# Attention in pairs of heads: score products on row halves of the array instead of stacked queries

## The chip, the cores and the metric

The kernel runs on one core of a Trainium2 chip. The metric is the device time of one execution in microseconds, the median of several runs. All stages stand in one program; engines are TensorE (PE in the profile, PEld for its loads of weights), VectorE (DVE), ScalarE (ACT), GpSimd (POOL) and SyncE (SP, which here only issues DMAs).

## The reference

Three stages, the output of each the input of the next: attention with a window of 128 keys and 4 sink keys (4 batches, 8 heads, 768 positions, head size 64); an expert-like layer over 3072 tokens (512 to 2048 to 512, with `h - tanh(h)` between); and a top-1 mixture of eight experts. Cut to the first, which the change is in, and the second, which shares its time:

```python
def _attn_ref(q, k, v, n_sink, window):
    scores = scale * np.matmul(q, k.transpose(0, 1, 3, 2))
    keep = is_sink | in_window
    scores = np.where(keep, scores, -1000000000.0)
    scores = scores - np.max(scores, axis=-1, keepdims=True)
    a = np.exp(scores)
    a = a / (np.sum(a, axis=-1, keepdims=True) + 1e-09)
    return np.matmul(a, v).astype(np.float32)

def _moe_ref(x, w_in, w_out):
    h = x @ w_in
    g = h - np.tanh(h)
    return (g @ w_out).astype(np.float32)
```

## The kernel before

**Tiling.** The 3072 tokens are cut into eight chunks of 384 (`NC`, three blocks of 128 queries, `TPC`). Two chunks are one batch. In a chunk the eight heads are four pairs (`HP`), and a pair of one chunk is a group `g`, 32 in all. A unit is one head and one query block: six in a group, 24 in a chunk, 192 in all. Each float32 operand is split into a float16 high and low part, and products are made of the parts.

**One unit.** `scores` makes two products of 128 rows by 128 queries by 260 keys (previous block, four sinks, own block; 132 in the first block of a batch). The stationary operand is `q_stack`, low queries on partitions 0 to 63 and high ones on 64 to 127; the moving one is first `kl_stack`, then `kh_stack`, which hold the low and high keys twice, on both halves of the partitions. Both accumulate in one bank, `s_ps` (the bank `acc0` for every second unit of the first chunk). VectorE adds the mask and takes the maximum (L585), ScalarE takes exponentials with their sum (L590), VectorE adds and inverts the sum (L602, L603), ScalarE scales (L608, `normed`). `transpose_probs` turns the two 128-column blocks with two transposes of float32 (L645) into one of two banks `pt_ps`; ScalarE takes the high part (L628) and VectorE the low part (L632). After each sixth unit `gather_sinks` and `transpose_sinks` do so for the sink columns of all six. After every second unit `weigh_values` multiplies with the values: the two heads of the pair write partitions 0 to 63 and 64 to 127 of one bank, `x_out`, with products of 64 columns of the array each (L707). After the sixth, `split_x` moves `x_out` into `xt_hi` (ScalarE) and `xt_lo` (VectorE).

**Conversions of a group.** `load_qk` loads each group's queries and keys twice, once to each half of the partitions. `qk_top_of` takes the largest magnitude (VectorE), `qk_scales` works out a power of two from it (eight small instructions, each behind the last), `qk_multiply` scales (GpSimd), `conv` makes the high part (ScalarE) and the low part (GpSimd, VectorE for the first group).

**The order of work** is written out by hand. `alone` runs the first 28 units, with the preparation of the weights beside them (`prepare_alone`). Then come eight windows of 32 slots, one window per chunk. Even slots make the hidden product of the next column block (`mlp_in`, twelve products of 384 columns, into `h_ps`), odd ones the output product (`mlp_out`, nine of 512 columns). ScalarE and VectorE do `tanh` (L762), `mlp_gate` (L771), `mlp_split` (L781) and `mlp_rest` (L791) for it. In each slot that is not a rest, one unit of attention of a later chunk has its scores and the transposes of the unit two before in the middle of the expert products (`between`), and the value products behind them. A product of `mlp_in` waits until `mlp_gate` has read `h_ps`. The router of the previous chunk (`gate_slot`) and the preparation of values of the next batch lie in fixed slots as well. After the windows the mixture of experts runs (`join`), with nothing of attention. TensorE executes in this order and waits in it.

## Time and profile before

| what | value |
|---|---|
| median of 3 runs | 1069.73 us (1068.58 to 1070.42) |
| profiled execution, span | 1067.3 us |
| TensorE busy | 986.2 us (92%) |
| VectorE busy | 699.5 us (66%) |
| ScalarE busy | 612.0 us (57%) |
| GpSimd busy | 400.9 us (38%) |
| first expert product | 90.4 us |
| windows 1 to 8 start at | 90.4, 180.0, 263.6, 353.3, 438.0, 527.6, 612.2, 696.7 us |

The span is that of one profiled execution. Busy is the union of an engine's instructions; matmuls overlap each other, so their mean duration is longer than their distance. The distance of two starts tells what one costs.

### The profile page before, as it was taken

Reading aid. Unit: us, or ns where it says so; the run is one execution under the profiler, and the core shown is the slowest. Engines: PE = TensorE matmul, PEld = TensorE weight load, DVE = VectorE, ACT = ScalarE, POOL = GpSimd, SP = SyncE. Lnnn points to the kernel's source line nnn. Section 1 sums busy time; section 2 is a strip of 40 time slices with the busy share of each in tenths; the row PEclk is TensorE's granted clock in tenths of the full one; section 3 lists DMA queues with packets and bytes.
Section 4 is the critical chain, followed back from the end, with each engine's and each line's share of the span. In section 5 each row is a group of like instructions: output and inputs, shape, how many; then the busy total and the mean of one; then the engine's idle time right before and its main releaser. Section 6 shows DMA issues by size and latency. Waiting matters only on the chain.

```text
span 1067.3 us, 24226 instructions
## 1 busy us (share of the span) xinstructions
PE 986.2 (92%) x7776; PEld 624.8 (59%) x7776; DVE 699.5 (66%) x2464; ACT 612.0 (57%) x1425; POOL 400.9 (38%) x462
## 2 busy tenths in 40 slices
PE   1668999999999999999899999999899999899996
PEld 0534555655565565556466556555487777677773
DVE  6677977668978867877876885637665334733331
ACT  2677887757766866767676776536412224522221
POOL 4788898213344412325522341011122322232322
PEclk9767999999999999999999999999999999999998
DMA  8943113311411333211231130051025111111111
GB/s 237 328 130 71 36 36 77 120 36 37 100 36 36 65 97 71 66 36 36 40 97 36 36 65 2 1 188 31 9 43 207 53 49 44 39 41 49 49 49 38
DMA packets 25165, 75.22 MB, mean 70 GB/s; under 512 B 10032, under 2 KB 10416, under 8 KB 23536
## 3 DMA queue, kind: packets, MB, share of 16 engines
q1 hardware_dynamic: 16176, 60.65, 21.1%
q0 software_dynamic: 5728, 13.43, 3.9%
q8 instruction: 44, 0.72, 0.3%
q10 hardware_dynamic: 3168, 0.02, 0.2%
q14 instruction: 49, 0.40, 0.1%
HBM read 60.23 MB, written 14.12 MB: 70 GB/s over the span
## 4 chain that ended last, share of the span: by engine, by line
PE 64%; DVE 19%; issue 5%; ACT 5%; DMA 3%; POOL 2%; DVEq 1%; SPq 1%; ACTq 0%; POOLq 0%
PE h_ps L750 16%; PE acc L806 15%; PE pt_ps L1846 10%; PE h_ps L1897 5%; PE acc L1897 5%; DVE qk_top L400 3%; DVE g_raw L771 2%; PE x_out L707 2%; PE pt_ps L645 2%; PE s_ps L575 2%; PE s_ps L857 2%; DVE pt_lo L632 1%; DVE g_lo L791 1%; DMA qk_raw<-in_qk 1%; DVE ew_lo L1542 1%
## 5 line engine op out<-in xcount | busy, mean ns | idle before, releaser
L806 PE MATMUL acc<-w_out_all,g_hi 128*128 128x512 f16 x768 | 228.4, 379 | 0.0
L750 PE MATMUL h_ps<-xt_hi,w_in_all 128*128 128x384 f16 x960 | 196.7, 328 | 14.7 <-DVE g_raw L771 14.6
L806 PE MATMUL acc<-w_out_all,g_lo 128*128 128x512 f16 x384 | 145.8, 380 | 4.6 <-DVE g_lo L791 2.8
L750 PEld LDWEIGHTS h_ps<-xt_hi,w_in_all 128*128 128x128 f16 x960 | 91.7, 98 | 84.2 <-DVE g_raw L771 18.9
L628 ACT ACTIVATE pt_hi<-pt_ps 128x256 f16<-128x256 f32 (+1 forms) x192 | 69.1, 360 | 114.3 <-PE pt_ps L645 113.6
L100 POOL TENSOR_TENSOR tick<-tick 1x1 f32<-1x1 f32 x83 | 16.0, 193 | 276.2 <-ACT y L1913 118.3
L806 PEld LDWEIGHTS acc<-w_out_all,g_hi 128*128 128x128 f16 x768 | 75.0, 98 | 70.2
L791 DVE SCALAR_TENSOR_TENSOR g_lo<-g_raw,batch_scale,g_hi 128x384 f16<-128x384 f32 x128 | 90.0, 703 | 34.9 <-ACT g_hi L781 33.5
L451 POOL TENSOR_TENSOR q_stack<-qk_raw,q_stack 64x768 f16<-64x768 f32 x31 | 51.1, 1650 | 164.3 <-ACT q_stack L447 164.3
L781 ACT ACTIVATE g_hi<-g_raw,batch_scale 128x384 f16<-128x384 f32 x128 | 78.1, 610 | 39.4 <-DVE g_raw L771 39.3
L608 ACT ACTIVATE normed<-probs,row_sum 128x260 f32<-128x260 f32 (+1 forms) x192 | 92.8, 484 | 12.0 <-DVE row_sum L603 11.6
L750 PE MATMUL h_ps<-xt_lo,w_in_all 128*128 128x384 f16 x480 | 98.3, 328 | 0.0
L762 ACT ACTIVATE g_raw<-h_ps,batch_scale 128x384 f32<-128x384 f32 x120 | 69.6, 580 | 49.1 <-PE h_ps L750 46.8
L771 DVE SCALAR_TENSOR_TENSOR g_raw<-h_ps,batch_scale,g_raw 128x384 f32<-128x384 f32 x120 | 73.5, 612 | 34.8 <-ACT g_raw L762 33.6
L590 ACT ACTIVATE probs<-probs,neg_max 128x260 f32<-128x260 f32 (+1 forms) x192 | 92.8, 483 | 2.8 <-DVE neg_max L585 2.8
L451 POOL TENSOR_TENSOR kl_stack<-qk_raw,kh_stack 128x1048 f16<-128x1048 f32 (+1 forms) x31 | 60.6, 1954 | 81.4 <-ACT kh_stack L447 81.3
L632 DVE TENSOR_TENSOR pt_lo<-pt_ps,pt_hi 128x256 f16<-128x256 f32 (+1 forms) x192 | 76.8, 400 | 20.0 <-ACT pt_hi L628 19.0
L645 PE MATMUL pt_ps<-ident,normed 128*128 128x128 f32 x352 | 75.5, 291 | 15.4 <-ACT normed L608 15.4
L585 DVE CUSTOM_DVE_ANT_0 probs<-s_ps,mask 128x260 f32<-128x260 f32 (+1 forms) x180 | 73.2, 407 | 24.5 <-issue 23.4
L1846 PE MATMUL pt_ps<-xg_hi,ew_lo 128*128 128x128 f16 x800 | 78.0, 220 | 0.0
L1846 PE MATMUL pt_ps<-xg_lo,ew_hi 128*128 128x128 f16 x800 | 78.0, 220 | 0.0
L1846 PE MATMUL pt_ps<-xg_hi,ew_hi 128*128 128x128 f16 x800 | 77.8, 220 | 0.0
(310 smaller groups left out, 2109.0 us busy)
## 6 DMA issues: line engine op xcount, KB each, us to landing
qk_raw<-in_qk SPq DMA_DIRECT2D x62, 454.0 KB, 6.0
raw<-in_w SPq DMA_DIRECT2D x16, 512.0 KB, 7.9
v_raw<-in_v SPq DMA_DIRECT2D x4, 1536.0 KB, 9.2
x_tokens<-x SPq DMA_DIRECT2D x24, 256.0 KB, 5.7
w_in_all<-in_w_in SPq DMA_DIRECT2D x4, 1024.0 KB, 13.0
w_out_all<-in_w_out SPq DMA_DIRECT2D x4, 1024.0 KB, 12.0
x_tokens<-g_raw SPq DMA_DIRECT2D x1, 1024.0 KB, 13.7
qk_raw<-in_qk SPq DMA_DIRECT2D x2, 262.0 KB, 4.4
```

The lines of the kernel that those rows point to most:

```text
L451: eng.tensor_tensor(lo, raw[half], hi[half], ALU.subtract).then_inc(q["conv_lo"], 1)
L590: eng.activation(probs[:, r, cols], probs[:, r, cols], ACT.Exp, bias=neg_max[:, r:r + 1], scale=-1.0, accum_out=row_sum[:, r:r + 1]).then_ ...
L608: eng.activation(normed[:, u % 6, cols], probs[:, r, cols], ACT.Copy, scale=row_sum[:, r:r + 1])\
L632: eng.tensor_tensor(pt_lo[:, at, :], out, pt_hi[:, at, :], ALU.subtract).then_inc(q["pt_lo_done"], 1)
L645: mm = eng.transpose(out[:, b, :], normed[:, u % 6, b * KB:b * KB + P], ident[:])
L750: mm = eng.matmul(h_of(m, f), w16[0][:, f, x * DM + k * P:x * DM + (k + 1) * P], r[:, par, k, :], start=(i == 0), stop=(i == 3 * KD - 1))
L771: eng.scalar_tensor_tensor(g, h_of(m, f), batch_scale[:, b, 0:1], g, ALU.mult, ALU.subtract).then_inc(q["g_done"], 1)
L781: eng.activation(g_hi[f % 2][:], g, ACT.Copy, scale=batch_scale[:, b, 1:2]).then_inc(q["g_hi_done"], 1)
L791: eng.scalar_tensor_tensor(g_lo[f % 2][:], g, batch_scale[:, b, 1:2], g_hi[f % 2][:], ALU.mult, ALU.subtract)\
L806: mm = eng.matmul(acc[t][:, :], l[f % 2][:, t * P:(t + 1) * P], w16[1][:, f, x * DM:(x + 1) * DM], start=(f == 0 and i == 0), stop=(f == N ...
L1846: mm = eng.matmul(hid_ps[c][:, (f - 4 * c) * P:(f - 4 * c + 1) * P], w[:, k, f * P:(f + 1) * P], x[p][:, k * P:(k + 1) * P], start=(i == 0 ...
L1897: mm = eng.matmul(y_ps[bank][:, :], l[:, f * P:(f + 1) * P], rhs, start=(f == 0 and i == 0), stop=(f == KF - 1 and i == 2))
```

## The change

The two heads of a pair lie side by side on the partitions (one on 0 to 63, one on 64 to 127), and a unit of work is a pair of heads with one query block: 96 pairs for 192 units.

- `qk_raw`, and in place of the stacks `q_hi`, `q_lo`, `k_hi`, `k_lo`, hold each number once; loads, tops, multiplies and conversions have half the elements per partition.
- `score_pair` makes eight products of 64 rows: for each of low by low, low by high, high by low and high by high, one on each row half, each half into its own bank (`s_ps0`, `s_ps1`). The eighth bank comes from the transposes, which have one bank `pt_ps` now, with both heads' four blocks in it. `h_of` takes `s_ps1` in the last window.
- Evacuations of the transposed blocks are one instruction of 512 elements for a pair. Masking, exponentials, sums and scaling stay one per head.
- The ring of `probs` has two pairs instead of three units.
- The order: a pair is scored in an even slot (`plan_slots` lists which), transposed in the even slot two later, its sinks (third block only) transposed three later, its values weighed three later (first and second block, odd slot) or four later (third block, even slot), and `split_x` five later, at the end of the odd slot. `alone` has 14 pairs. The router's transposes and logits come one slot earlier.

Its core:

```diff
-    qk_raw = [sb(f"qk_raw{s}", [P, 2, QK], F32) for s in range(2)]
-    q_stack = [sb(f"q_stack{s}", [P, 2, CT], F16) for s in range(2)]
-    kh_stack, kl_stack = ([sb(f"k{x}_stack{s}", [P, 2, KR], F16) for s in range(2)] for x in ("h", "l"))
+    qk_raw = [sb(f"qk_raw{s}", [P, QK], F32) for s in range(2)]
+    q_hi, q_lo = ([sb(f"q_{x}{s}", [P, CT], F16) for s in range(2)] for x in ("hi", "lo"))
+    k_hi, k_lo = ([sb(f"k_{x}{s}", [P, KR], F16) for s in range(2)] for x in ("hi", "lo"))
...
-                for j, k in enumerate((kl_stack, kh_stack)):
-                    mm = eng.matmul(bank[:, cols], q_stack[s][:, hh, t * P:(t + 1) * P],
-                                    k[s][:, hh, t * KB + cols.start:t * KB + KW], start=(j == 0), stop=(j == 1))
+                claim_scores(eng, (q["shifted"], 2 * r + 1))
+                need(eng, q["shifted"], 2 * r)
+                for i, (l, k) in enumerate(((q_lo, k_lo), (q_lo, k_hi), (q_hi, k_lo), (q_hi, k_hi))):
+                    for j in range(2):
+                        rows = slice(D * (1 - j), D * (2 - j))
+                        mm = eng.matmul(s_banks[j][:, cols], l[s][rows, t * P:(t + 1) * P],
+                                        k[s][rows, t * KB + cols.start:t * KB + KW], start=(i == 0), stop=(i == 3))
...
+        def transpose_probs(E, eng, r):
...
+            out = pt_bank[:].rearrange("p (j b c) -> p j b c", j=2, b=2)[:, :, first:2, :]
+            free = pv_count(TPC * (g - 1) + (1, 2, 2)[t])
...
+                need(eng, q["pt_lo_done"], m)
+                for j in range(2):
+                    for b in range(first, 2):
+                        mm = eng.transpose(out[:, j, b - first, :], normed[:, 2 * t + j, b * KB:b * KB + P], ident[:])
...
+                begins = t == (0 if a % 2 else 1)
                 if begins:
-                    need(eng, q["xt_lo_done"], v)
+                    need(eng, q["xt_lo_done"], g)
...
+            for r in range(ALONE):
                 if E == "pe":
+                    stage(score_pair, E, eng, r)
+                    stage(transpose_probs, E, eng, r - 1)
+                    stage(weigh_values, E, eng, r - 2, True)
                 if E == "act":
+                    stage(score_pair, E, eng, r)
+                    stage(transpose_probs, E, eng, r - 1)
+                    stage(split_x, E, eng, r - 2)
                 if E == "dve":
+                    stage(score_pair, E, eng, r)
+                    stage(gather_sinks, E, eng, r - 1)
+                    stage(transpose_probs, E, eng, r - 1)
...
+                if E == "pe":
+                    if r in (4, 8):
+                        weight_spread(E, eng, r // 8)
+                    stage(transpose_sinks, E, eng, r - 1)
+                    stage(weigh_values, E, eng, r - 1, False)
...
+            for w in range(NC):
+                for k in range(0, SLOTS, 2):
+                    if k not in ((10, 20, 30) if w == 0 else (4, 10, 16, 26)):
+                        scored[SLOTS * w + k] = r
+                        r += 1
...
                     def between():
-                        stage(scores, E, eng, n)
-                        stage(transposes, E, eng, n - 2)
+                        if even:
+                            stage(score_pair, E, eng, ago(0))
+                            stage(transpose_probs, E, eng, ago(2))
+                        else:
+                            stage(transpose_sinks, E, eng, ago(3))
                     if not even:
                         mlp_out(E, eng, w, f, between)
+                        stage(weigh_values, E, eng, ago(3), False)
+                    else:
+                        if nxt:
+                            mlp_in(E, eng, *nxt, between)
+                        stage(weigh_values, E, eng, ago(4), True)
                 if E == "act":
                     if even:
-                        stage(transposes, E, eng, n - 2)
+                        stage(transpose_probs, E, eng, ago(2))
                         if nxt:
                             mlp_in(E, eng, *nxt)
+                        stage(score_pair, E, eng, ago(0))
                     else:
                         if nxt:
                             mlp_split(E, eng, *nxt)
+                        stage(normalise, E, eng, ago(1))
+                        stage(transpose_sinks, E, eng, ago(3))
+                        stage(split_x, E, eng, ago(5))
                 if E == "dve":
+                    if even:
+                        stage(score_pair, E, eng, ago(0))
+                        stage(gather_sinks, E, eng, ago(2))
+                        stage(transpose_probs, E, eng, ago(2))
+                    else:
+                        if nxt:
+                            mlp_gate(E, eng, *nxt)
+                        stage(normalise, E, eng, ago(1))
+                        if nxt:
+                            mlp_rest(E, eng, *nxt)
+                        stage(transpose_sinks, E, eng, ago(3))
+                        stage(split_x, E, eng, ago(5))
```

## Rows read from the trace of the kernel before

**Rows 1.** The page: busy time of the engines, GB/s in 40 slices, loads of queries and keys
```profile
PE 986.2 (92%) x7776; PEld 624.8 (59%) x7776; DVE 699.5 (66%) x2464; ACT 612.0 (57%) x1425; POOL 400.9 (38%) x462
...
GB/s 237 328 130 71 36 36 77 120 36 37 100 36 36 65 97 71 66 36 36 40 97 36 36 65 2 1 188 31 9 43 207 53 49 44 39 41 49 49 49 38
...
qk_raw<-in_qk SPq DMA_DIRECT2D x62, 454.0 KB, 6.0
```

**Rows 2.** Busy time by stage: PE, PEld, DVE, ACT, POOL, clock, DMA, GB/s
```profile
0.00:90.40 90.40, 45.49 (x322) 29.26 (x322) 63.77 (x270) 55.93 (x147) 65.31 (x83) 0.76 0.70 215
...
263.60:353.30 89.70, 86.08 (x583) 50.85 (x582) 74.86 (x268) 63.82 (x158) 39.91 (x35) 1.00 0.23 52
353.30:438.00 84.70, 83.09 (x554) 49.47 (x553) 64.50 (x253) 58.52 (x151) 24.72 (x21) 1.00 0.30 73
```

**Rows 3.** TensorE's waits from 90.4 to 696.7 us: total, times, longest
```profile
PE h_ps L750 <- DVE g_raw L771: 14.6, 20, 1.8
PE s_ps L575 <- DVE neg_max L585: 1.9, 3, 0.8
PE acc L806 <- POOL w_out_all L361: 1.5, 1, 1.5
```

**Rows 4.** TensorE in order of time: start us, busy us, line, tile
```profile
401.25 0.81 PE L750 MATMUL h_ps<-xt_lo,w_in_all 128*128 128x384 f16 x4
401.90 0.81 PE L750 MATMUL h_ps<-xt_hi,w_in_all 128*128 128x384 f16 x4
...
406.57 0.81 PE L750 MATMUL h_ps<-xt_hi,w_in_all 128*128 128x384 f16 x4
407.31 0.30 PE L707 MATMUL x_out<-pt_lo,v_hi 128*64 128x256 f16 x2
407.44 0.28 PE L707 MATMUL x_out<-pt_hi,v_lo 128*64 128x256 f16 x2
407.55 0.28 PE L707 MATMUL x_out<-pt_hi,v_hi 128*64 128x256 f16 x2
407.76 1.06 PE L857 MATMUL s_ps<-w_gate,x2t 128*128 128x8 f32 x8
...
412.58 0.27 PE L575 MATMUL s_ps<-kl_stack,q_stack 128*128 128x260 f16 x1
412.69 0.27 PE L575 MATMUL s_ps<-kh_stack,q_stack 128*128 128x260 f16 x1
```

**Rows 5.** Instructions of the whole run by line, VectorE then ScalarE: busy us, mean ns
```profile
L632 DVE TENSOR_TENSOR pt_lo<-pt_ps,pt_hi 128x256 f16<-128x256 f32 x160 | 67.5, 422 | 17.8 <-ACT pt_hi L628 16.9
L585 DVE CUSTOM_DVE_ANT_0 probs<-s_ps,mask 128x260 f32<-128x260 f32 x152 | 64.9, 427 | 16.1 <-issue 15.0
...
L400 DVE TENSOR_REDUCE qk_top<-qk_raw 128x1 f32<-128x1048 f32 x16 | 19.8, 1237 | 0.1
...
L730 DVE SCALAR_TENSOR_TENSOR xt_lo<-x_out,xt_hi 128x384 f16<-128x384 f32 x32 | 17.6, 549 | 0.3
...
L608 ACT ACTIVATE normed<-probs,row_sum 128x260 f32<-128x260 f32 x160 | 80.2, 501 | 8.7 <-DVE row_sum L603 8.3
L590 ACT ACTIVATE probs<-probs,neg_max 128x260 f32<-128x260 f32 x160 | 80.2, 501 | 0.0
L781 ACT ACTIVATE g_hi<-g_raw,batch_scale 128x384 f16<-128x384 f32 x128 | 78.1, 610 | 39.4 <-DVE g_raw L771 39.3
L762 ACT ACTIVATE g_raw<-h_ps,batch_scale 128x384 f32<-128x384 f32 x120 | 69.6, 580 | 49.1 <-PE h_ps L750 46.8 <-issue 0.9
...
L727 ACT ACTIVATE xt_hi<-x_out 128x384 f16<-128x384 f32 x32 | 15.7, 490 | 0.8 <-PE x_out L709 0.7
```

**Rows 6.** GpSimd's subtractions for queries and keys, whole run: busy us, mean ns
```profile
L451 POOL TENSOR_TENSOR q_stack<-qk_raw,q_stack 64x768 f16<-64x768 f32 x31 | 51.1, 1650 | 164.3 <-ACT q_stack L447 164.3
L451 POOL TENSOR_TENSOR kl_stack<-qk_raw,kh_stack 128x1048 f16<-128x1048 f32 x16 | 34.9, 2179 | 39.8 <-ACT kh_stack L447 39.8
```

**Rows 7.** The chain that ended last: start us, us, what
```profile
17.91 11.17 DMA vs_raw<-in_v
```

More of the change, by code:

```diff
@@ L39 @@
 HP = H // 2
-UPC = TPC * H
+PPC = TPC * HP
+PAIRS = NC * PPC
 SLOTS = 2 * NF
@@ L564, in scores, with is_first, span, pv_count @@
+        def is_first(r):
+            return r // PPC % 2 == 0 and r % TPC == 0
+        def span(r):
+            return slice(P if is_first(r) else 0, KW)
+        def pv_count(r):
+            return sum(not is_first(i) for i in range(r + 1))
+        def turned(r):
+            return (TPC + 1) * (r // TPC) + r % TPC
+        def score_pair(E, eng, r):
+            a, t, hp, g = place(r)
             s = g % 2
-            cols = span(n)
-            bank = acc[0] if a == 0 and u % 2 else s_bank
+            cols = span(r)
@@ L611, in gather_sinks @@
[L611 to L615 removed]
+                for j in range(2):
+                    x = probs[:, r % RING, j, cols]
+                    eng.wait_ge(q["shifted"], 2 * r + j + 1)
+                    eng.activation(x, x, ACT.Exp, bias=neg_max[:, r % RING, j:j + 1], scale=-1.0,
+                                   accum_out=row_sum[:, r % RING, j:j + 1]).then_inc(q["exped"], 1)
@@ new lines, in normalise @@
+        def normalise(E, eng, r):
+            a, t, hp, g = place(r)
+            cols = span(r)
+            for j in range(2):
+                n = 2 * r + j
+                total = row_sum[:, r % RING, j:j + 1]
+                if E == "dve":
+                    step = chain(eng, q["inverted"], 2 * n)
+                    eng.wait_ge(q["exped"], n + 1)
+                    step(eng.tensor_scalar(total, total, 1e-9, DOWN, ALU.add, ALU.mult))
+                    eng.reciprocal(total, total).then_inc(q["inverted"], 1)
+                if E == "act":
+                    eng.wait_ge(q["inverted"], 2 * n + 2)
+                    if j == 0:
+                        need(eng, q["transposed"], turned(r) - TPC)
+                        need(eng, q["sink_copied"], g)
+                    eng.activation(normed[:, 2 * t + j, cols], probs[:, r % RING, j, cols], ACT.Copy, scale=total)\
+                       .then_inc(q["normal"], 1)
@@ L616, in gather_sinks @@
+        def gather_sinks(E, eng, r):
+            a, t, hp, g = place(r)
+            if E == "dve" and t == TPC - 1:
+                need(eng, q["transposed"], (TPC + 1) * g)
                 if g == 0:
@@ L1272, in window, with plan_slots @@
+                prepare_alone(E, eng, 2 * r + 1)
+                conversions(E, eng, 2 * r + 1)
+        scored = {2 * (r - ALONE): r for r in range(ALONE)}
+        def plan_slots():
+            r = ALONE
+            for w in range(NC):
[3 more added lines that the diff above has]
+                        r += 1
+        def window(E, eng, w):
             for k in range(SLOTS):
@@ L1310, in window @@
-                    stage(scores, E, eng, n)
-                    stage(transposes, E, eng, n - 2)
-                    stage(sinks_of_pair, E, eng, n - 1)
-                    if nxt and not even:
-                        mlp_rest(E, eng, *nxt)
+                    if even:
[10 more added lines that the diff above has]
+                        stage(split_x, E, eng, ago(5))
```

314 lines of the change are left out of this document (115 added, 199 removed).

## Prediction

> **What bounds the kernel now.** I read the page first, for the shares of the engines [rows 1]: TensorE is busy for 986 of 1067.3 us, VectorE for 700, ScalarE for 612, GpSimd for 401. An average hides stages, so the busy time by stage comes next [rows 2]. The reader is to see two regimes there. In the 90.4 us before the first expert product (the stage of `alone`) TensorE works for 45 us only, while VectorE, ScalarE and GpSimd each work for 56 to 65: nothing is saturated, and a loop of hand-overs between engines sets the pace. In the windows behind it TensorE works 86 of 89.7 us and 83 of 84.7: there the time is TensorE's own, and another engine matters only where TensorE waits for it. So the third view is what TensorE waits for between 90.4 and 696.7 us [rows 3]: 14.6 + 1.9 + 1.5 us, and 0.2 more, 18.2 us in 606, nearly all of it for VectorE's `g_raw` (the bank `h_ps` is not free yet). This is the cap on what lighter VectorE, ScalarE and GpSimd work can give in the windows. Whatever is added to TensorE's own sequence there counts in full. Behind 696.7 us nothing of attention is left, and that stage I leave as it is.
>
> **TensorE's sequence: the price of the half rows.** I count columns streamed. A unit (one head, one query block) now has two products of all 128 rows, the stacked [low; high] queries against high and against low keys; a pair of heads has four. After it a pair has eight products of 64 rows, four on each row half. If two halves run side by side, the streaming time is that of four again. Start to start, a 260-column product takes 0.11 us (412.58 to 412.69 [rows 4]), so a pair costs 0.44 us before and 0.44 after; if they don't run side by side, 0.88.
> The trace of before has no product on row halves. The nearest rows are the value products L707, which use column halves: six products of 256 columns start in three couples at 407.31, 407.44 and 407.55 [rows 4], 0.12 us a couple. One after the other they would take over 0.2. So halves of the array do work side by side in this kernel, and I take that for the rows too. The couples write different banks (`s_ps0`, `s_ps1`), so they don't meet in one.
> The same rows show what leaving the full array costs. Expert products L750 follow each other at 0.1625 us (401.25 to 401.90 for four). Four that start at 406.57 are thus streamed by 407.22, and the first half-array product starts at 407.31: 0.09 us late. The last couple starts at 407.55, is streamed by 407.66, and the next full product starts at 407.76: 0.10 us late. The score products before have no such gap (412.58, 412.69, in step with their neighbours). In and out is **0.19 us**, and the change adds one such round trip per pair, as the scores stand between expert products L750 and full transposes. The value products keep theirs, one per pair in both kernels. In the windows 82 pairs are scored (13 in the first, 12 in five, 9 in the last): 82 x 0.19 = **15.6 us** on the critical engine. Bounds: 0 us if row halves need no such gap, which no row excludes, and 0.25 us a pair (20.5 us) if a 128-column load of weights shows behind the switch where a 64-column one does now. I take 0.19, the only gap of the kind that the trace has.
> A rule of the Trainium skill (TensorEngine Tiling (Array Packing), Key Properties) bears on this: changing the tiling mode, not just the tile, drains the engine. The gaps of 0.09 and 0.10 us around L707 agree with it. It speaks against this change, since it would hold for rows as for columns.
>
> **What gets lighter.** Each group of six units (`g`) converts queries and keys that are no longer kept twice. The reduction `qk_top` goes from 768 and 1048 elements per partition to 384 and 524 (1.24 us for 1048 [rows 5], so about 0.65 after, 1.1 us less per `g` together). GpSimd's subtractions go from 1.65 and 2.18 us [rows 6] to about half, 1.9 us less per `g`, its multiplies and ScalarE's conversions likewise. Loads of queries and keys halve. The transposed probabilities of both heads are evacuated by one instruction of 512 elements for two of 256: 0.42 us each now [rows 5], about 0.69 after (256 more elements at the rate that 1.24 us per 1048 gives, near 1 ns each), so 0.15 us less per pair on VectorE. Row sums, softmax, exponents and normalising keep their number. VectorE gains some 0.15 + 1.1/3 = 0.5 us per pair, against about 5.5 us that two slots take, and it was the engine waited for in [rows 3]. I count 13 of these 18.2 us as gone, with bounds of 5 and 18: waits are shorter than 2 us each, and half a microsecond of lead per pair plus the early place of `mlp_gate` in its slot removes most but not those where the tops of values, the scale exponents and the router fall in one slot. **-13 us.**
>
> **What the new order adds.** `score_pair` and `transpose_probs` lie in even slots, the sinks' transposes and the value products in odd ones, the value products of the third block one even slot later. I follow `x_out`, since it is a single bank. For an odd chunk, the third block's products of one head pair end an even slot, and the next pair's first block comes at the end of the very next odd slot, after `mlp_out`; in between `split_x` on both engines must have emptied the bank, and `split_x` stands last in that odd slot on ScalarE and VectorE. With 0 at the start of the even slot: TensorE has its third-block products done by 3.85, `mlp_out` (nine products of 0.216) by 5.8, and wants the bank then. ScalarE does tanh from 3.0 (0.58), the two exponentials (0.50 plus a read of 0.19 that overlaps, about 0.65 each) to 4.9, `g_hi` 0.61 to 5.5, two times `normed` 0.50 to 6.5, `xt_hi` 0.49 to 7.0, and VectorE `xt_lo` 0.55 to 7.6 [rows 5]. TensorE waits about 1.8 us. Before, two whole slots lay between the same two steps. From the slot lists this adjacency comes twelve times in the windows; in five of them both slots are full (1.8 to 2.4 us), in seven a slot without a pair lies beside it and ScalarE is early (0.4 us). 5 x 1.8 + 7 x 0.4 = **+12 us**, bounds 3 (ScalarE ahead of this plan) and 20. With one transpose bank for two, the sinks' transposes wait for `pt_lo` of the pair; that is done at 3.9 and wanted at 4.3, so I count nothing, and 0.4 us for each of 28 groups (11 us) if VectorE is late: it is within the bound of 20.
>
> **The stage alone.** Its start is lighter: the sinks' load, on which GpSimd and the scores of the fourth pair hang, lands at 29.1, 11.2 us after its issue [rows 7]. Loads come in at 237 GB/s in the first 26.7 us, and queries and keys are 2 x 454 KB per `g`, three times up to there [rows 1]; half of these 2.7 MB fall away, 1.36 MB or some 5 us, and the first conversions are half as long. Then the pace. Now the stage goes from 36.4 to 90.4 us for 10.75 pairs, 5.0 us a pair. After it, one pair on VectorE: two score evictions (0.51 each), a wait for ScalarE's two exponentials and the evacuation to about 2.3, `pt_lo` 0.7, the row sums of two heads 0.7, so 3.7 us, and a third of sinks, `x_out`, tops and exponents (1.3): 5.0 us. ScalarE's exponentials stand ahead of the evacuation, so the loop is more serial, and that eats what the conversions give. The pace stays. **-4 us**, between -12 (if the gain of the conversions counts too) and +6 (TensorE ran below its full clock in that stage, 0.76 on the mean [rows 2], and now closes the loop within a pair).
>
> **Sum.** 15.6 - 13 + 12 - 4 = +10.6 us on the span of 1067.3 us. The three runs have a median of 1069.7, 2.4 us above the profiled execution, so 1067.3 + 10.6 + 2.4 = **1080.3 us**.
>
> **Rivals.**
> (a) The row halves don't run side by side: 4 x 0.11 x 82 = 36 us more, 1116 us. For it: no row shows them. Against it: the column halves do. Another rule of the skill (TensorE: Matmul & The Clock Gate, Part 3) says that products on distinct row groups start within 4 ns of each other; no row of before shows that. Chance 0.1.
> (b) The other side: row halves go in and out of the full array without a gap, as the full products do among themselves. Then 15.6 us fall out, 1064.7 us, faster. It decides where a round trip costs under 0.035 us (12.7 us less over 82 pairs). For it: the gap at L707 could belong to columns alone, whose weights are 64 wide. Against it: both sides of L707 show it. Chance 0.13.
> (c) The x_out wait and the stage alone come out at their good ends (3 and -12) while the waits for `g_raw` go: 15.6 - 15 + 3 - 10 = -6, 1063 to 1070 us. Here the lighter engines pay for the switches. For it: VectorE's 64 us of 90 in the stage alone, which include all that halves. Against it: the serial loop worked out above. Chance 0.17.
> (d) The order costs more than planned, x_out and the single transpose bank at 20 us and the stage alone at +3: 1095 us. Chance 0.1.
> The forecast's own case holds 0.5, with a range from 1072 to 1090 us.
>
> **Chances and range.** A change of 0.2% is 2.1 us, about what a measurement of this kernel can tell from none. Below 1067.6: all of (b) but a little and most of (c), 0.24. Between 1067.6 and 1071.9: 0.1. Above: 0.66. The range leaves out (a) and the very lowest of (b): 1062 to 1098 us.
>
> **What would show it.** Start to start around the score products, 0.25 us instead of 0.16 from the last L750 to the first of them and 0.21 instead of 0.11 from the last to the transposes; couples 0.11 us apart. TensorE's waits in the windows: `g_raw` down to about 5 us, a new row of `x_out` waiting for `xt_lo`, some 12 us in twelve waits. The first expert product at 86 instead of 90.4 us. POOL busy some 80 us less. If the first window alone is shorter than 89.6 us, or no wait at `x_out` shows, my picture of the order is wrong.

## The result and the profile after

The changed kernel takes 1111.47 us (1111.31 to 1112.77, four runs) against 1070.08 us of the kernel before: a ratio of 1.0392, 95% interval 1.037 to 1.0413. The forecast of 1080.3 us had the direction and a quarter of the size, and the time lies above its range. Its profiled execution has a span of 1111.2 us, 43.9 us more than the one before.

The page: busy time of the engines, then GB/s in slices.

```profile
PE 1010.6 (91%) x8160; PEld 616.7 (55%) x8160; DVE 650.9 (59%) x2272; ACT 580.8 (52%) x1329; POOL 328.4 (30%) x462
...
GB/s 297 253 34 17 18 19 35 103 18 19 62 1 35 46 76 19 20 60 18 18 64 18 18 46 2 1 13 197 1 31 98 151 47 47 52 31 55 48 48 37
...
qk_raw<-in_qk SPq DMA_DIRECT2D x31, 454.0 KB, 3.4
```

What was to get lighter did: VectorE works 49 us less than in [rows 1], ScalarE 31, GpSimd 72, and the loads of queries and keys are half as many. TensorE works 24 us more, and on balance none of the lighter engines' time comes back.

Busy time by stage (stage, its length, then PE, PEld, DVE, ACT, POOL, clock, DMA share, GB/s), the stages as in [rows 2]: before the first expert product, the first window, the third and the fourth.

```profile
0.00:89.80 89.80, 44.78 (x385) 29.67 (x385) 54.06 (x251) 53.31 (x140) 59.12 (x86) 0.80 0.50 181
89.80:191.60 101.80, 89.69 (x597) 46.75 (x595) 67.98 (x235) 68.87 (x163) 60.39 (x67) 0.94 0.07 21
...
278.50:375.30 96.80, 90.66 (x625) 50.26 (x625) 67.53 (x244) 59.90 (x146) 30.34 (x35) 0.98 0.13 29
375.30:464.70 89.40, 86.71 (x608) 48.30 (x608) 59.25 (x230) 54.33 (x139) 15.76 (x21) 1.00 0.19 49
```

The first stage ends 0.6 us earlier (90.4 before). The seven windows with attention take 649.6 us for 606.3: all of the loss, 43.3 us, lies there. The window of 89.7 us in [rows 2] now takes 96.8, with 6.1 us in which TensorE isn't busy, for 3.6.

TensorE's waits in these windows (total, times, longest), to be held against [rows 3]:

```profile
PE x_out L707 <- issue: 15.6, 12, 2.5
PE h_ps L752 <- DVE g_raw L773: 12.6, 23, 1.6
PE pt_ps L641 <- DVE pt_hi L673: 6.3, 13, 0.9
```

Two new rows, 15.6 us in 12 waits for `x_out` and 6.3 us in 13 for the transposes' bank (VectorE writes the low part of the sinks into the tile `pt_hi`, L673), and the old one for `g_raw` is hardly smaller, 12.6 for 14.6 us. The view gives `issue` as the releaser of the first; the timeline below names the real one.

TensorE in order of time around one pair:

```profile
471.76 0.81 PE L752 MATMUL h_ps<-xt_lo,w_in_all 128*128 128x384 f16 x4
472.50 0.28 PE L571 MATMUL s_ps<-k_lo,q_lo 64*128 64x260 f16 x2
472.62 0.27 PE L571 MATMUL s_ps<-k_hi,q_lo 64*128 64x260 f16 x2
472.74 0.27 PE L571 MATMUL s_ps<-k_lo,q_hi 64*128 64x260 f16 x2
472.85 0.28 PE L571 MATMUL s_ps<-k_hi,q_hi 64*128 64x260 f16 x2
473.05 0.66 PE L641 MATMUL pt_ps<-ident,normed 128*128 128x128 f32 x4
473.54 0.65 PE L752 MATMUL h_ps<-xt_hi,w_in_all 128*128 128x384 f16 x3
```

Each score line is a couple (x2), one product per row half, and couples follow at 0.11 to 0.12 us, as one full product did in [rows 4]. Four expert products from 471.76 are streamed at 472.41, and the first couple starts at 472.50; the last is streamed at 472.96, and the transposes start at 473.05. By single records, over all windows, the step into the row halves is 0.258 us instead of 0.162, and out of them 0.202 instead of 0.108: 0.096 + 0.094 = 0.190 us. One thing more shows there. Four transposes of 0.109 us would be through at 473.49; the next product starts at 473.54. The first transpose behind the row halves takes 0.165 us (median of 49), and 0.109 where a full product stands ahead of it.

One wait for `x_out`, on three engines:

```profile
482.37 0.59 PE L808 MATMUL acc<-w_out_all,g_hi 128*128 128x512 f16 x2
...
482.72 0.61 ACT L783 ACTIVATE g_hi<-g_raw,batch_scale 128x384 f16<-128x384 f32 x1 [0.97 <-DVE g_raw L773]
483.24 0.90 ACT L609 ACTIVATE normed<-probs,row_sum 128x260 f32<-128x260 f32 x2
484.04 0.47 ACT L729 ACTIVATE xt_hi<-x_out 128x384 f16<-128x384 f32 x1
...
484.54 0.56 DVE L732 SCALAR_TENSOR_TENSOR xt_lo<-x_out,xt_hi 128x384 f16<-128x384 f32 x1 [0.56 <-ACT xt_hi L729]
...
485.20 0.25 PE L707 MATMUL x_out<-pt_lo,v_hi 128*64 128x128 f16 x2 [2.24 <-issue]
```

`mlp_out` is streamed by 482.8; ScalarE makes `g_hi`, both `normed`, and only then `xt_hi`; VectorE ends `xt_lo` at 485.10, and at 485.20 the value products start, after 2.24 us of idle time.

### The profile page after: what moved, and what is told of

Same layout as the page of the kernel before. It is cut to its first block, busy times and chain, and to the rows that moved or that the text cites. A ratio compares the mean times of both kernels' runs of the same rounds, so it can differ in the third digit from the quotient of the medians.

```text
span 1111.2 us, 24223 instructions
## 1 busy us (share of the span) xinstructions
PE 1010.6 (91%) x8160; PEld 616.7 (55%) x8160; DVE 650.9 (59%) x2272; ACT 580.8 (52%) x1329; POOL 328.4 (30%) x462
## 4 chain that ended last, share of the span: by engine, by line
PE 66%; DVE 14%; issue 9%; ACT 8%; DMA 2%; DVEq 1%; POOL 0%; ACTq 0%; SPq 0%; POOLq 0%
PE h_ps L752 17%; PE acc L808 14%; PE h_ps L1909 5%; PE s_ps L1858 5%; PE pt_ps L1858 5%; PE acc L1909 5%; PE pt_ps L641 4%; PE s_ps L571 3%; PE x_out L707 2%; ACT probs L589 2%; DVE g_raw L773 2%; DVE pt_lo L650 2%; PE s_ps L859 1%; ACT pt_hi L646 1%; ACT normed L609 1%
## 5 line engine op out<-in xcount | busy, mean ns | idle before, releaser
L752 PE MATMUL h_ps<-xt_hi,w_in_all 128*128 128x384 f16 x960 | 198.6, 330 | 12.6 <-DVE g_raw L773 12.6
L101 POOL TENSOR_TENSOR tick<-tick 1x1 f32<-1x1 f32 x83 | 15.6, 188 | 318.4 <-DVE payload L931 129.6
L650 DVE TENSOR_TENSOR pt_lo<-pt_ps,pt_hi 128x512 f16<-128x512 f32 (+1 forms) x96 | 62.1, 647 | 69.8 <-ACT pt_hi L646 59.8
L582 DVE CUSTOM_DVE_ANT_0 probs<-s_ps,mask 128x260 f32<-128x260 f32 (+1 forms) x192 | 70.0, 402 | 51.3 <-issue 41.6
L646 ACT ACTIVATE pt_hi<-pt_ps 128x512 f16<-128x512 f32 (+1 forms) x96 | 53.6, 558 | 81.8 <-PE pt_ps L641 81.5
L609 ACT ACTIVATE normed<-probs,row_sum 128x260 f32<-128x260 f32 (+1 forms) x192 | 83.1, 480 | 11.0 <-DVE row_sum L602 9.0
L641 PE MATMUL pt_ps<-ident,normed 128*128 128x128 f32 x352 | 62.5, 300 | 14.8 <-ACT normed L609 8.4
L450 POOL TENSOR_TENSOR q_lo<-qk_raw,q_hi 128x384 f16<-128x384 f32 x31 | 28.3, 914 | 130.1 <-ACT q_hi L446 130.1
L752 PEld LDWEIGHTS h_ps<-xt_lo,w_in_all 128*128 128x128 f16 x480 | 47.8, 100 | 32.7 <-issue 2.5
L1822 ACT ACTIVATE xg<-xg,x_scale 128x512 f32<-128x512 f32 x23 | 16.6, 722 | 93.3 <-DVE x_undo L1819 93.3
L429 POOL TENSOR_SCALAR qk_raw<-qk_raw,qk_scale 128x384 f32<-128x384 f32 (+2 forms) x62 | 40.0, 656 | 79.0 <-DVE qk_scale L420 79.0
L641 PEld LDWEIGHTS pt_ps<-ident,normed 128*128 128x128 f32 x352 | 40.4, 149 | 37.1 <-issue 21.0
## 6 DMA issues: line engine op xcount, KB each, us to landing
w_out_all<-in_w_out SPq DMA_DIRECT2D x4, 1024.0 KB, 10.6
```

The costliest lines, as they stand in the source:

```text
L582: eng.tensor_tensor_reduce(out=probs[:, r % RING, j, cols], in0=s_banks[j][:, cols], in1=m, scale=-SCALE, scalar=3.0e38, op0=ALU.add, op1= ...
L609: eng.activation(normed[:, 2 * t + j, cols], probs[:, r % RING, j, cols], ACT.Copy, scale=total)\
L641: mm = eng.transpose(out[:, j, b - first, :], normed[:, 2 * t + j, b * KB:b * KB + P], ident[:])
L650: eng.tensor_tensor(at(pt_lo), out, at(pt_hi), ALU.subtract).then_inc(q["pt_lo_done"], 1)
L752: mm = eng.matmul(h_of(m, f), w16[0][:, f, x * DM + k * P:x * DM + (k + 1) * P], r[:, par, k, :], start=(i == 0), stop=(i == 3 * KD - 1))
```

## The experiments

All change one thing in the changed kernel, unless said otherwise. Times are medians. Ratios are to the kernel before, measured beside each run on the same chip, with a 95% interval. The last column is the difference by these ratios, in us.

| run | median us | ratio | against | by ratio |
|---|---|---|---|---|
| x_early | 1094.96 | 1.0243 (1.0196 to 1.0290) | changed -16.5 | -15.9 |
| sinks_early | 1101.16 | 1.0301 (1.0251 to 1.0351) | changed -10.3 | -9.7 |
| scales_odd | 1096.69 | 1.0273 (1.0229 to 1.0317) | changed -14.8 | -12.7 |
| alone_evac | 1100.88 | 1.0312 (1.0249 to 1.0375) | changed -10.6 | -8.5 |
| full_rows | 1093.18 | 1.0226 (1.0160 to 1.0293) | changed -18.3 | -17.7 |
| one_half | 1139.53 | 1.0674 (1.0624 to 1.0724) | changed +28.1 | +30.1 |
| before_trip | 1082.10 | 1.0123 (1.0073 to 1.0173) | before +12.6 | +13.1 |
| all_order | 1065.51 | 0.9979 (0.9964 to 0.9994) | changed -46.0 | -44.1 |
| beside | 1064.27 | 0.9972 (0.9958 to 0.9986) | all_order -1.2 | -0.7 |
| order_full | 1050.07 | 0.9829 (0.9805 to 0.9852) | all_order -15.4 | -16.0 |
| before_scales | 1066.13 | 0.9976 (0.9963 to 0.9989) | before -2.3 | -2.6 |

The kernel before took 1070.08 us beside the changed kernel, 1069.48 beside `x_early`, `sinks_early`, `full_rows` and `before_trip`, 1067.68 beside `scales_odd`, `alone_evac`, `one_half` and `all_order`, and 1068.42 beside the last three, so a plain difference of medians can be 2 us off. The single changes and `before_trip` have two executions each, and intervals of some 5 to 7 us to each side. That of `alone_evac` just meets that of the changed kernel (1.0249 to 1.0375, and 1.037 to 1.0413); its effect rests on the trace.

My theory after the result: the cost has two parts, the round trips to the row halves, which nothing hides, and places in the written order, each of which makes TensorE wait though no engine is full. The rival: ScalarE and VectorE are too loaded in full slots, and a wait removed at one place comes back at another.

**x_early.** In the odd slot, `split_x` comes first on ScalarE and behind `mlp_gate` on VectorE.

```diff
                     else:
+                        stage(split_x, E, eng, ago(5))
                         if nxt:
                             mlp_split(E, eng, *nxt)
                         stage(normalise, E, eng, ago(1))
                         stage(transpose_sinks, E, eng, ago(3))
-                        stage(split_x, E, eng, ago(5))
...
                             mlp_gate(E, eng, *nxt)
+                        stage(split_x, E, eng, ago(5))
                         stage(normalise, E, eng, ago(1))
                         if nxt:
                             mlp_rest(E, eng, *nxt)
                         stage(transpose_sinks, E, eng, ago(3))
-                        stage(split_x, E, eng, ago(5))
```

> The changed kernel with split_x moved forward in the odd slot: first on ScalarE, directly behind mlp_gate on VectorE. Theory (the place of split_x makes TensorE wait 17.8 us for x_out): these waits fall to 1 to 4 us and the time by 10 to 17 us, to about 1097 us. Rival (ScalarE and VectorE are simply loaded too much in these slots, so the wait moves to g_raw or normed): x_out falls, g_raw and normed rise by the same, time within 4 us of 1111.

Measured -16.5 us. Waits in the windows:

```profile
PE h_ps L752 <- DVE g_raw L773: 13.5, 21, 1.7
PE pt_ps L641 <- DVE pt_hi L673: 6.4, 13, 0.9
PE x_out L707 <- issue: 1.4, 4, 0.5
```

`x_out` falls from 15.6 to 1.4 us, and the other rows keep their size (12.6 to 13.5, 6.3 to 6.4). The wait was one of place. The two stretches at half clock that follow two of these waits in the changed kernel (last section) are not there either; how much of the gain is theirs isn't separated.

**sinks_early.** `transpose_sinks` ahead of `normalise` on ScalarE, in the odd slot.

```diff
-                        stage(normalise, E, eng, ago(1))
                         stage(transpose_sinks, E, eng, ago(3))
+                        stage(normalise, E, eng, ago(1))
                         stage(split_x, E, eng, ago(5))
```

> The changed kernel with ScalarE's evacuation of the sinks' transposes ahead of normalise in the odd slot. Theory (one transpose bank: TensorE's transposes of the next pair wait for the sinks' low part, 6.3 us of idle time in 13 waits and some 9 us start to start): the waits fall by 4 to 6 us and the time by 4 to 8 us. Rival (the wait only moves on to normed or g_raw): within 2 us of 1111.

Measured -10.3 us, more than the 4 to 8 expected. The wait in question, in the changed kernel, on three engines:

```profile
477.67 0.47 ACT L669 ACTIVATE pt_hi<-pt_ps 128x384 f16<-128x384 f32 x1
...
478.17 0.55 DVE L673 TENSOR_TENSOR pt_hi<-pt_ps,pt_hi 32x384 f16<-32x384 f32 x1 [0.56 <-ACT pt_hi L669]
...
478.86 0.63 PE L641 MATMUL pt_ps<-ident,normed 128*128 128x128 f32 x4 [0.39 <-DVE pt_hi L673]
```

ScalarE takes the sinks out of the one bank behind both `normed`, VectorE follows, and only then may TensorE write the next pair's transposes. This wait falls from 6.3 us in 13 to:

```profile
PE pt_ps L641 <- DVE pt_hi L673: 1.8, 4, 0.6
```

That is 4.5 us of idle time in a gain of 10.7 us over the windows. Start to start the transposes' delay falls by some 6 us, as each of the nine waits that are gone counts about 0.17 us more than its idle gap (see the sum below). The clock gives more. The changed kernel has two stretches at half clock in the middle of its windows (last section), worth 3.4 us, and this one has none there; and its TensorE is back at 2.4 GHz at 92.8 us, the changed kernel's only at 98.2. The pieces come to more than the gain, so they aren't separated to a microsecond.

**scales_odd.** From group 5 on (counted from 0), the chain of eight small VectorE instructions of `qk_scales` goes to the end of the odd slot, behind `mlp_gate`; GpSimd's order stays.

```diff
-                if i == tops[2]:
+                if i == tops[2] + (g >= 5):
                     qk_scales(E, eng, *at)
+                if i == tops[2]:
                     qk_multiply(E, eng, *at)
```

> The changed kernel with the chain of eight small VectorE instructions for the scales of queries and keys (from the fifth group on) one slot later, behind mlp_gate and at the end of an odd slot. Theory (the waits for g_raw come from this chain, which stands ahead of mlp_gate in the queue): the 12.6 us of waits for g_raw in the windows fall by 4 to 8 us and the time by 3 to 8 us. Rival (other work is late as well, or the next evictions of scores pay for it): within 2 us.

Measured -14.8 us, or -12.7 by the ratios; both are more than the 3 to 8 expected. Waits in the windows:

```profile
PE x_out L707 <- issue: 15.4, 12, 2.5
...
PE h_ps L752 <- DVE g_raw L773: 2.3, 3, 1.6
```

`g_raw` falls from 12.6 to 2.3 us, `x_out` stays. So this one chain in front of `mlp_gate` made four fifths of the wait that I had expected lighter work to remove. The rest of the gain is not separated: 20 waits fewer count 0.17 us each beyond their idle gap, the two half-clock stretches are absent in this profile too, and its first stage ends 1.9 us earlier; against that stand 2.2 us of new waits of the sinks' transposes for `pt_lo`. The chain's first and last instruction in the changed kernel, `mlp_gate` behind it, and the expert products that wait:

```profile
469.00 0.14 DVE L412 TENSOR_SCALAR qk_exp<-qk_top 128x1 int32<-128x1 int32 x1
...
470.36 0.15 DVE L420 TENSOR_SCALAR qk_scale<-qk_scale 128x1 int32<-128x1 int32 x1
470.43 0.61 DVE L773 SCALAR_TENSOR_TENSOR g_raw<-h_ps,batch_scale,g_raw 128x384 f32<-128x384 f32 x1
...
471.10 0.82 PE L752 MATMUL h_ps<-xt_hi,w_in_all 128*128 128x384 f16 x4 [0.80 <-DVE g_raw L773]
```

The chain holds VectorE from 469.00 to 470.51, and TensorE, free at 470.3, starts at 471.10.

**alone_evac.** In the stage alone, ScalarE evacuates the transposed probabilities of the last pair ahead of the exponentials of this one.

```diff
+                    stage(transpose_probs, E, eng, r - 1)
                     stage(score_pair, E, eng, r)
-                    stage(transpose_probs, E, eng, r - 1)
```

> The changed kernel with ScalarE's evacuation of the transposed probabilities ahead of the exponentials in the stage alone. Theory (that stage gains nothing because VectorE waits there for two exponentials and the evacuation): the first expert product comes at 78 to 84 instead of 89.8 us, the time falls by 5 to 11 us. Rival (TensorE's own order or the loads of the weights set the pace): within 2 us.

Measured -10.6 us; the first expert product comes at 81.5 us. VectorE's `pt_lo` in that stage (busy, mean | idle before it), in the changed kernel and then in this one:

```profile
L650 DVE TENSOR_TENSOR pt_lo<-pt_ps,pt_hi 128x512 f16<-128x512 f32 (+1 forms) x13 | 7.9, 609 | 17.7 <-ACT pt_hi L646 17.7
```

```profile
L650 DVE TENSOR_TENSOR pt_lo<-pt_ps,pt_hi 128x512 f16<-128x512 f32 (+1 forms) x13 | 7.9, 608 | 8.5 <-ACT pt_hi L646 8.4
```

17.7 us of waiting for ScalarE become 8.5. This order is not new: in the kernel before, ScalarE's evacuation already stands ahead of its exponentials in `alone`, and the change had turned the two round.

**full_rows and before_trip**: the price of the round trip, once taken away and once added. `full_rows` has four products of 128 rows per pair:

```diff
-                for i, (l, k) in enumerate(((q_lo, k_lo), (q_lo, k_hi), (q_hi, k_lo), (q_hi, k_hi))):
-                    for j in range(2):
-                        rows = slice(D * (1 - j), D * (2 - j))
-                        mm = eng.matmul(s_banks[j][:, cols], l[s][rows, t * P:(t + 1) * P],
-                                        k[s][rows, t * KB + cols.start:t * KB + KW], start=(i == 0), stop=(i == 3))
+                for j in range(2):
+                    for i, (l, k) in enumerate(((q_lo, k_hi), (q_hi, k_hi))):
+                        mm = eng.matmul(s_banks[j][:, cols], l[s][:, t * P:(t + 1) * P],
+                                        k[s][:, t * KB + cols.start:t * KB + KW], start=(i == 0), stop=(i == 1))
```

> The changed kernel with four score products of all 128 rows per pair (two per bank) in place of eight of 64 rows: the same streaming, no change between half rows and full array. The scores then mix both heads, so this is not attention; only its time counts. Theory (0.19 us per round trip): the gaps of 0.258 and 0.202 us around the scores become 0.162 and 0.111, and the time falls by 13 to 17 us, less if the waits for x_out take up the freed time. Rival (the round trips are absorbed by the waits): under 5 us.

Measured -18.3 us (-17.7 by the ratios), a little more than the 13 to 17 expected, and -18.8 in the windows: 82 x 0.190 = 15.6, and 49 x 0.056 = 2.7 for the first transpose behind the scores, which takes 0.109 us here. That fits to half a microsecond, and by some luck: it has two half-clock stretches too, but leaves the half clock of the start at 90.6 us instead of 98.2, which alone can be worth up to 3 us.

`before_trip` adds to the kernel before:

```diff
+                if u % 2 == 0:
+                    eng.matmul(s_bank[:, 504:508], q_stack[s][D:P, hh, t * P:(t + 1) * P],
+                               kh_stack[s][D:P, hh, t * KB + cols.start:t * KB + cols.start + 4], start=True, stop=True)
```

> The kernel before with one tiny product of 64 rows and 4 columns per pair, into unused columns of s_ps, ahead of the scores of every second unit: a round trip to the half rows per pair, nothing else. Theory: 0.19 us plus about 0.03 for the product, 82 times in the windows, so 15 to 19 us slower than before, 1085 to 1089 us. Rival (hidden in waits): under 8 us.

Measured +12.6 us, less than expected. TensorE around it:

```profile
412.71 0.81 PE L753 MATMUL h_ps<-xt_lo,w_in_all 128*128 128x384 f16 x4
413.46 0.17 PE L575 MATMUL s_ps<-kh_stack,q_stack 64*128 64x4 f16 x1
413.57 0.23 PE L578 MATMUL s_ps<-kl_stack,q_stack 128*128 128x132 f16 x1
```

A product of four columns takes 0.2 us of TensorE's time, 0.096 to get in (413.36 to 413.46) and 0.107 with the product itself to get out. That is 16.6 us for 82, but the waits for `g_raw` fall from 14.6 to 11.2 us: the kernel before has waits that a trip can hide in, and the windows grow by 12.8.

**one_half.** All eight score products on the lower row half.

```diff
-                        rows = slice(D * (1 - j), D * (2 - j))
+                        rows = slice(0, D)
```

> The changed kernel with the eight score products all on the lower row half, into the same two banks, so none can run beside another. The scores of both heads are those of one, only the time counts. Theory (the row halves do run side by side in the changed kernel): 4 x 0.11 us more for each of 82 pairs, 30 to 38 us slower than the changed kernel, near 1145 us. Rival (they did not): no difference.

Measured +28.1 us (+30.1 by the ratios), at or just under the bottom of what I expected. The products of one half follow each other singly:

```profile
485.91 0.39 PE L571 MATMUL s_ps<-k_lo,q_lo 64*128 64x260 f16 x2
486.14 0.38 PE L571 MATMUL s_ps<-k_hi,q_lo 64*128 64x260 f16 x2
486.36 0.38 PE L571 MATMUL s_ps<-k_lo,q_hi 64*128 64x260 f16 x2
```

Two now take 0.22 us, where a couple took 0.11: the row halves of the changed kernel do run side by side, and rival (a) is excluded, though its 1116 us came closest to the time. It is less than 36 us for two reasons: 12 of the 82 pairs have products of 132 columns, which leaves some 33 us, and TensorE's waits in the windows fall from 35.1 to 30.4 us.

**all_order**: the four edits of the order together.

> The changed kernel with all four edits of the order: split_x first, sinks evacuated early, scales one slot later, evacuation ahead of the exponentials in alone. Theory: the single gains add, 16.5 + 10.3 us and what scales_odd and alone_evac give (8 to 15 us together), so 1070 to 1080 us; what is left over the kernel before is the round trips to the half rows. Rival (the waits feed each other and move on to g_raw): 1085 us or more.

Measured 1065.51 us, -46.0 against the changed kernel (-44.1 by the ratios), 0.21% below the one before (eight runs), and less than the 1070 to 1080 expected. By the ratios the single gains would add to 47, so most of each stays. Waits from 80 to 700 us, the rows over 1 us:

```profile
PE pt_ps L664 <- DVE pt_lo L650: 2.2, 4, 0.6
PE h_ps L752 <- DVE g_raw L773: 1.6, 1, 1.6
PE x_out L707 <- issue: 1.4, 4, 0.5
```

The rival falls: with the same instructions on the same engines, nearly all waits are gone. Its windows take 615.0 us, 8.7 more than before, and the first expert product comes at 80.0 us, 10.4 earlier.

**order_full**: `all_order` with the score products of `full_rows`.

> all_order with four full-array score products per pair (both heads mixed, not attention, only the time counts). Theory (with the waits gone, what the round trips cost stands alone: 0.096 + 0.094 us and 0.056 us at the first transpose behind them): 16 to 20 us less than all_order, 1046 to 1050 us. Rival (they are partly hidden by waits): under 12 us.

Measured 1050.07 us, -15.4, or -16.0 by the ratios, at the lower edge of the 16 to 20 that I gave. The windows are 14.9 us shorter, and TensorE's waits in them rise from 6.5 to 8.2 us. With most waits gone, the round trips and the slower transposes behind them cost some 1.5% of the kernel; without them the pair layout would be 1.7% below the kernel before.

**beside**: `all_order` with the value products between the scores and the transposes, in even slots.

```diff
                             stage(score_pair, E, eng, ago(0))
+                            if (w, k) != (0, 0):
+                                stage(weigh_values, E, eng, ago(4), False)
+                            stage(weigh_values, E, eng, ago(4), True)
                             stage(transpose_probs, E, eng, ago(2))
...
                         mlp_out(E, eng, w, f, between)
-                        stage(weigh_values, E, eng, ago(3), False)
...
                             mlp_in(E, eng, *nxt, between)
-                        stage(weigh_values, E, eng, ago(4), True)
```

> all_order with the value products moved between the score products and the transposes, all in even slots four slots behind their scores: full array to row halves to column halves to full array, three changes in place of four. Theory (each change of the array's division costs 0.09 to 0.1 us, whichever way): 82 x 0.095 = 7.8 us less, and up to 3 us more where the transposes' extra 0.056 us behind row halves goes too, so 1055 to 1059 us. Rival (row halves to column halves costs as much as both changes through the full array): 1063 to 1067 us.

Measured 1064.27 us, -1.2 (-0.7 by the ratios), which the noise does not tell from none and which would fit the rival as well. The trace decides between the two. From row halves straight to column halves:

```profile
401.22 0.22 PE L571 MATMUL s_ps<-k_hi,q_hi 64*128 64x132 f16 x2
401.37 0.36 PE L707 MATMUL x_out<-pt_lo,v_hi 128*64 128x256 f16 x4
```

The last couple of 132 columns (0.055 us) is streamed by 401.28, and the value products start 0.09 us later: the change from rows to columns costs what one change to the full array does, and not two (0.093 us, median over the windows). So the price was right and the count was wrong. In the trace the value products stand directly behind scores 46 times; the others fall into slots without scores, and first blocks of a batch have none of their own. 46 x 0.093 = 4.3 us. The windows are 2.3 us shorter, and TensorE's waits in them rise from 6.5 to 10.1 us. Nor do the transposes get their 0.056 us back: the first one behind column halves takes 0.165 us too (median of 28).

**before_scales.** The kernel before, with the same chain moved behind `mlp_gate` where it stood at the end of an even slot.

```diff
...
                 if i == tops[2]:
-                    qk_scales(E, eng, *at)
+                    if g >= 5 and k is not None and k % 2 == 0:
+                        late.append(at)
+                    else:
+                        qk_scales(E, eng, *at)
                     qk_multiply(E, eng, *at)
...
+                if late and not even:
+                    qk_scales(E, eng, *late.pop())
```

> The kernel before with the same edit as scales_odd: where the chain of eight small VectorE instructions falls at the end of an even slot, it goes to the end of the odd slot behind it, and so behind mlp_gate. Theory (this wait is a matter of the order, not of the change): waits for g_raw fall from 14.6 to 6 to 9 us in the windows, the time to 1060 to 1065 us. Rival (the kernel before waits for other things): no change.

Measured 1066.13 us, -2.3, less of a gain than I expected. `g_raw` falls from 14.6 to 7.1 us, but the scores' waits rise:

```profile
PE h_ps L750 <- DVE g_raw L771: 7.1, 12, 1.6
PE s_ps L575 <- DVE neg_max L585: 3.6, 5, 0.8
```

In the kernel before part of the wait does move on. Why is argued, not shown: its single scores are evicted one slot behind each other. `beside` and `before_scales` were measured side by side, 1064.27 and 1066.13 us, with ranges that overlap. Whether the pair layout in its best order beats the kernel before in a better order is thus not settled; both beat the kernel before by 0.2 to 0.3%. They do it in different places: the windows take 612.7 us in `beside` and 602.9 in `before_scales`, and the first expert product comes at 79.1 and 90.5 us.

## Why the prediction was right or wrong

**Streaming and round trips: right.** The couples run side by side, their two products starting 3 to 4 ns apart, and the way in and out costs 0.190 us for the 0.19 read at the value products. The Trainium skill's rule that a change of the tiling mode drains the engine (TensorEngine Tiling (Array Packing), Key Properties) agrees with the traces, by gaps of 0.093 to 0.107 us, for rows, for columns and from rows straight to columns. The extra 0.056 us at the first transpose was not seen coming; with it a pair whose transposes stand right behind its scores pays 0.246 us, at the upper bound. Taken away alone it is 18.3 us.

**x_out: right in mechanism and count, short in size.** Twelve adjacencies were counted from the slot lists, twelve waits came: 15.6 us for 12, and 16.5 us when the cause is taken away, the clock that it brings included. The five long waits are 10.1 us for 9.0 (1.5 to 2.5 each for 1.8), and the seven short ones 5.5 for 2.8 (0.8 each for 0.4): most of the miss is there. In the wait shown above, ScalarE's `g_hi` starts 0.1 us ahead of the end of `mlp_out`, where the plan had 0.9, behind a VectorE that first takes tops of values and of queries and only then does the gate (VectorE ahead of that wait):

```profile
480.76 0.68 DVE L477 TENSOR_REDUCE v_top<-v_raw 128x1 f32<-128x512 f32 x1
481.47 0.56 DVE L401 TENSOR_REDUCE qk_top<-qk_raw 128x1 f32<-128x384 f32 x1
482.06 0.62 DVE L773 SCALAR_TENSOR_TENSOR g_raw<-h_ps,batch_scale,g_raw 128x384 f32<-128x384 f32 x1
```

**The single transpose bank: the step failed.** I asked whether the sinks' transposes find the bank empty, and they do. I did not ask whether the next pair's transposes do, behind the sinks' own low part, last in the odd slot but one. That is 6.3 us of idle time in 13 waits, where I had put nothing, and 10.3 us of the kernel when it goes (the clock included). "I count nothing" had a bound of 11 us, which held.

**-13 us for lighter engines: the step failed**, and it is the largest miss: the rows of [rows 3] shrank by 5 us, not 13. The waits of [rows 3] were taken for a lack of capacity on VectorE, so that half a microsecond less per pair would remove most. VectorE works 49 us less, and `g_raw` is still waited for 12.6 us. `scales_odd` shows why: one serial chain of 1.5 us stood directly ahead of `mlp_gate` in the queue. It is as long as before, since its eight dependent instructions work on one column each, 0.14 to 0.21 us in both kernels, whatever the size of the data.

**The stage alone: half right.** The start gains what was worked out: the fourth pair's scores begin at 31.1 us for 36.4, 5.3 us for the 5 from the loads. "The pace stays" was wrong: 58.7 us for 10.75 pairs, 5.46 us a pair for 5.0, and with it the term of -4 us came out at -0.6. The serial link that I had named, exponentials ahead of the evacuation, was already in my 5.0 us, but too cheap. `alone_evac` takes the link away: 51.9 us from 29.6 on, 4.8 us a pair. What my sum of 5.0 left out is not shown; TensorE's way back to the next scores in the half-clock stretches is my guess.

**The sum.** The forecast for the windows was 15.6 - 13 + 12 = 14.6 us. Measured were 43.3 us: 15.6 for the round trips, 3 for the first transposes behind them (56 of the 82 pairs have them there), 15.6 + 6.3 us of new waits, 4 because an idle gap is counted from the modelled end of a product, some 0.17 us after the next could have started (25 new waits), 3.4 for the clock, less 2.0 + 1.9 + 1.3 for the rows of [rows 3] that shrank. That makes 43; half a clock that lasts to 98.2 us instead of the 94.8 of before could add up to 2, so the account is good to some 2 us, no better. Of the rivals, (d) had the right mechanisms and was too cheap; (b) and (c) fell. In (c) the sum has -10 us for the stage alone where its condition says -12, which decides nothing.

## What to carry to other kernels

Count how often a sequence changes the division of the array, not only the columns: 0.19 us a round trip, on an engine without slack, was more than all that the lighter engines gave in the windows, which are 8.7 us longer than before even in `all_order`. Before a wait is put down to a loaded engine, look at what stands directly ahead of the awaited instruction in its queue; four moves of a line or two each were worth 44 to 46 us here, with the same instructions. And when steps are regrouped, check for each single bank who empties it and where in its queue that stands, for the next writer too.

## What the runs showed of the hardware

- The changes from full array to row halves, to column halves, back from either, and from row halves straight to column halves each cost 0.093 to 0.107 us, with one product of four columns as with eight of 260. From columns to rows was not measured.
- The first float32 transpose behind row halves takes 0.165 us instead of 0.109, and so does the first one behind column halves (nine of the router's in the changed kernel, 28 in `beside`). So it goes with the return to the full array, not with rows. Why isn't known.
- A wait can cost more than itself. After two of the waits for `x_out` (2.47 us at 117.9, 2.23 at 298.6) the granted clock went to 1.2 GHz for 3.4 us. Behind an equal one (2.24 us at 485.2) it did not. Expert products behind the second, four to a line:

```profile
298.57 0.25 PE L707 MATMUL x_out<-pt_lo,v_hi 128*64 128x128 f16 x2 [2.23 <-issue]
...
299.36 1.27 PE L752 MATMUL h_ps<-xt_hi,w_in_all 128*128 128x384 f16 x4
300.42 1.49 PE L752 MATMUL h_ps<-xt_lo,w_in_all 128*128 128x384 f16 x4
```

Four take 1.06 us there, from 299.36 to 300.42, for 0.65 in [rows 4]. Granted clock of that stretch and of the one after 117.9 (the third column from the end; 0.50 is 1.2 GHz):

```profile
299.60:303.00 3.40, 3.40 (x14) 2.08 (x13) 0.20 (x1) 0.75 (x2) 0.07 (x1) 0.50 0.45 137
118.70:122.10 3.40, 3.40 (x18) 1.66 (x16) 0.89 (x5) 0.00 (x0) 2.14 (x2) 0.50 0.13 16
```

Over all traces, such a stretch in the windows comes only at waits of this length. Six traces (the changed kernel, `alone_evac`, `full_rows`, `one_half`, `sinks_early`, `scales_odd`) have three waits of 2.2 to 2.5 us for `x_out` there. The first four show two half-clock stretches of 3.4 us each there, and all eight start between 0.2 us before and 1.0 us after the end of such a wait; `sinks_early` and `scales_odd` show none. The other seven traces have no wait over 1.9 us in their windows, and once the clock has risen there, it stays at 2.4 GHz. So 8 of 18 such waits cost the clock; which of them it will be isn't settled here. (The last stage, without attention, has such stretches of its own in some traces, the kernel before's at 777.5 us among them.)
